# Spare matmuls on zeros between attention levels, and a reordered start, in a fused recurrence and two-layer expert kernel

## What is computed

```python
for t in range(S):
    kt, vt, rt, wt = (k[:, :, t], v[:, :, t], r[:, :, t], w[:, :, t])
    cur = np.einsum('bhd,bhe->bhde', u[None] * kt, vt)
    y[:, :, t] = np.einsum('bhd,bhde->bhe', rt, state + cur)
    state = wt[:, :, :, None] * state + np.einsum('bhd,bhe->bhde', kt, vt)
...
h = x @ w_in
g = np.where(pos, h, np.where(neg, 0.0, (h + beta) ** 2 / (4.0 * beta)))   # layer 1
g = np.where(h > 0.0, h, alpha * (np.exp(np.minimum(h, 0.0)) - 1.0))       # layer 2
return (g @ w_out)
```

## Time and profile before

| | |
|---|---|
| median of 3 runs | 1022.77 us (1022.32 to 1023.42) |
| profiled execution, own time | 1023.31 us |
| its span (first to last instruction) | 1021.5 us |
| PE busy | 989.6 us, 97% |
| DVE / ACT / POOL busy | 554.2 / 517.4 / 46.7 us |
| chain that ended last | PE 90%, DVE 4%, POOL 2% |

### The profile page before, as it was taken

One profiled execution on the slowest core, in us unless ns is written; L12 is line 12 of the kernel. 1 busy time (PEld: TensorE's weight loads), 2 busy tenths in 40 slices (PEclk: granted clock), 3 DMA queues, 4 the chain that ended last, 5 costly groups with the idle time before them and its releaser, 6 DMA issues.

```text
span 1021.5 us, 25102 instructions
## 1 busy us (share of the span) xinstructions
PE 989.6 (97%) x11080; PEld 812.3 (80%) x11080; DVE 554.2 (54%) x824; ACT 517.4 (51%) x926; POOL 46.7 (5%) x44
## 2 busy tenths in 40 slices
PE   4799899999999999999999999999999999999998
PEld 4788888777777777787778888888888888888886
DVE  5687877667666766776643454433433333333332
ACT  3465356454635354545456775554445444444543
POOL 5830000000000000000000000000000000000000
PEclk9899999999999999999999999999999999999999
DMA  9622032032002203020206000000000001000000
GB/s 327 200 79 96 24 121 110 3 141 78 33 28 115 80 33 115 28 80 33 95 1 216 1 31 31 32 21 11 32 31 1 31 32 31 31 1 1 31 1 31
DMA packets 24699, 61.71 MB, mean 60 GB/s; under 512 B 2448, under 2 KB 6928, under 8 KB 24592
## 3 DMA queue, kind: packets, MB, share of 16 engines
q1 hardware_dynamic: 24592, 60.12, 16.7%
HBM read 50.68 MB, written 9.44 MB: 59 GB/s over the span
## 4 chain that ended last, share of the span: by engine, by line
PE 90%; DVE 4%; POOL 2%; issue 1%; ACT 1%; DMA 1%; SPq 0%; ACTq 0%; DVEq 0%; POOLq 0%
PE down_banks L576 39%; PE up_bank L576 29%; PE g_banks L576 17%; PE y_bank L576 3%; DVE att L1025 1%; POOL win_lo L515 1%; PE y_bank L628 1%; DMA scratch<-w_in_dram 1%; PE y_bank L710 1%; POOL r_nat L525 0%; DVE r_nat L1054 0%; DVE att L1007 0%; DVE att L1037 0%; DVE ynat L1075 0%; DVE ynat L1078 0%
## 5 line engine op out<-in xcount | busy, mean ns | idle before, releaser
L576 PE MATMUL down_banks<-g_hi,wout_lo 128*128 128x512 f32 (+1 forms) x624 | 246.1, 394 | 0.0
L576 PE MATMUL down_banks<-g_hi,wout_hi 128*128 128x512 f32 (+1 forms) x624 | 235.9, 378 | 0.0
L576 PE MATMUL down_banks<-g_lo,wout_hi 128*128 128x512 f32 (+1 forms) x624 | 235.5, 377 | 0.0
L821 ACT CAST g_hi<-scratch 128x512 fp32r<-128x512 f32 (+1 forms) x192 | 116.0, 604 | 188.8 <-PE down_banks L576 118.9
L1096 DVE TENSOR_TENSOR g_lo<-scratch,g_hi 128x512 fp32r<-128x512 f32 (+1 forms) x192 | 128.4, 669 | 108.6 <-ACT g_hi L821 107.0
L576 PE MATMUL up_bank<-x_hi,win_lo 128*128 128x512 f32 (+1 forms) x480 | 182.6, 380 | 3.0 <-DVE g_lo L1096 1.8
L576 PE MATMUL up_bank<-x_lo,win_hi 128*128 128x512 f32 (+1 forms) x480 | 179.5, 374 | 0.0
L576 PE MATMUL up_bank<-x_hi,win_hi 128*128 128x512 f32 (+1 forms) x480 | 179.4, 374 | 0.0
L576 PEld LDWEIGHTS down_banks<-g_hi,wout_lo 128*128 128x128 f32 x624 | 117.8, 189 | 23.6
L576 PEld LDWEIGHTS down_banks<-g_hi,wout_hi 128*128 128x128 f32 x624 | 117.9, 189 | 23.3
L576 PEld LDWEIGHTS g_banks<-att 64*64 64x64 f32 (+1 forms) x5184 | 105.5, 136 | 36.2 <-issue 20.5
(11 more groups left out here) (98 smaller groups left out, 1075.6 us busy)
## 6 DMA issues: line engine op xcount, KB each, us to landing
att<-rT_dram SPq DMA_DIRECT2D x12, 512.0 KB, 4.0
att<-kT_dram SPq DMA_DIRECT2D x12, 512.0 KB, 5.6
att<-wT_dram SPq DMA_DIRECT2D x12, 512.0 KB, 6.5
r_nat<-rN_dram SPq DMA_DIRECT2D x12, 384.0 KB, 6.7
k_nat<-kN_dram SPq DMA_DIRECT2D x12, 384.0 KB, 7.7
att<-vN_dram SPq DMA_DIRECT2D x12, 384.0 KB, 6.9
x_dram<-r_nat SPq DMA_DIRECT2D x18, 256.0 KB, 2.3
ynat<-x_dram SPq DMA_DIRECT2D x6, 768.0 KB, 4.3
```

Source lines behind the costliest of these rows:

```text
L576: return nc.tensor.matmul(out, lhsT, rhs, start=start, stop=stop, **kw)
L821: return nc.scalar.copy(out, in_)
```

## The change

Five things, all in the first 60 us of the program:

- TensorE: 16 spare matmuls on a zeroed tile (128 rows, 256 columns, float32r) ahead of level 0 of group 0, then 11, 11, 9, 9, 9, 9 and 4 after its seven levels, and 3, 5 and 8 around the two `turn_x`. They write a PSUM place that nobody reads until slot 1 overwrites it. VectorE clears the tile first.
- VectorE: in group 0 of chunk 0 the mask of level l - 1 comes after the update of level l.
- GpSimd: `times_keys(0)` and `times_bonus(0)` after three weight pieces instead of six, `diagonal_output(0)` after six instead of nine and without its wait for them, `times_keys(1)` behind it.
- Pieces 6 to 8 get a buffer of their own (`extra`) in place of `ynat`, so that `diagonal_output` may write `ynat` sooner and pieces 19 and 20 no longer wait for piece 8.
- ScalarE: a one-column copy right at the start. A scratch area of the transfers is made smaller (memory for `extra`).

```diff
-STAGE = ["g0", "g1", "q", "scores0", "scores1", "scores2", "y0", "y1", "y2",
+STAGE = ["g0", "g1", "q", "scores0", "scores1", "scores2", "extra0", "extra1", "extra2",
...
-STAGED_BEHIND = {**{i: 5 for i in range(9, 14)}, 18: 2, 19: 8, 20: 8, 22: 16, 23: 17, 24: 18, 25: 22, 26: 23, 27: 21}
+STAGED_BEHIND = {**{i: 5 for i in range(9, 14)}, 18: 2, 22: 16, 23: 17, 24: 18, 25: 22, 26: 23, 27: 21}
+IDLE_AFTER_LEVEL = (11, 11, 9, 9, 9, 9, 4)
...
+        extra = sb("extra", [P, 3, TOK])
...
+        table_loaded = sb("table_loaded", [P, 1])
+        idle_work = x_lo[1][:, 0, 0:TH]
...
-                pool.wait_ge(w1_lo_ready, 9 if g == 0 else 21)
+                if g == 1:
+                    pool.wait_ge(w1_lo_ready, 21)
...
-            for i in range(6):
+            for i in range(3):
                 lo_of_weights(i)
             times_keys(0)
             times_bonus(0)
-            times_keys(1)
-            for i in range(6, 9):
+            for i in range(3, 6):
                 lo_of_weights(i)
             diagonal_output(0)
-            for i in range(9, 14):
+            times_keys(1)
+            for i in range(6, 14):
                 lo_of_weights(i)
...
+            def keep_busy(n):
+
+                for _ in range(n):
+                    mm(up_bank[1][:, 0:TH], idle_work[:, 0:P], idle_work)
+
+            pe.wait_ge(idle_work_ready, 1)
+            keep_busy(16)
             for l in range(NL):
                 pair_products(0, 0, l)
+                keep_busy(IDLE_AFTER_LEVEL[l])
             for b in range(2):
                 attend(0, b)
             turn_k(0, 0)
-            for b in range(2):
-                turn_x(0, b)
+            keep_busy(3)
+            turn_x(0, 0)
+            keep_busy(5)
+            turn_x(0, 1)
+            keep_busy(8)
...
             act.wait_ge(consts_ready, 1)
+            copy(table_loaded[:, :], consts[:, 0:1])
...
+            nc.vector.memset(idle_work.bitcast(F32), 0.0).then_inc(idle_work_ready, 1)
...
                 update(0, 0, l)
-                mask(0, 0, l)
+                if l:
+                    mask(0, 0, l - 1)
                 next_decays(0, 0, l)
```

More of the change, by code:

```diff
@@ L139, in build @@
                    **{f"scores_{i}": a_[1][:, i * DM:(i + 1) * DM] for i in range(5)},
-                   **{f"y{i}": ynat_flat[:, i * TOK:(i + 1) * TOK] for i in range(3)},
+                   **{f"extra{i}": extra[:, i, :] for i in range(3)},
                    **{f"y_{i}": ynat_flat[:, (2 + i) * DM:(3 + i) * DM] for i in range(2)},
@@ L193, in build @@
         consts_ready = sem("consts_ready")
+        idle_work_ready = sem("idle_work_ready")
         scores_zeroed = [sem(f"scores_zeroed{g}") for g in range(2)]
@@ L1244 @@
     arrays = {n: np.ascontiguousarray(a) for n, a in arrays.items()}
-    nc = bacc.Bacc("TRN2", target_bir_lowering=False, num_devices=1)
+    nc = bacc.Bacc("TRN2", target_bir_lowering=False, num_devices=1, dynamic_dma_scratch_size=8192)
     args = [nc.dram_tensor(n + "_dram", a.shape, mybir.dt.from_np(a.dtype), kind="ExternalInput").ap()
```

## The result

Over all its runs the changed kernel took 1027.45 us (median; 1023.22 to 1030.27), the kernel before, on the same chips, 1023.11 us (1021.36 to 1025.73): a ratio of 1.0044, 95% interval 1.0033 to 1.0056. It is slower by 4.3 us, by more than the 0.2% that can be told from no change, and lies above the range of the prediction. The profiled execution took 1029.1 us with a span of 1027.3 us.

The account below looks back on a forecast made before the run. The first 52 us decide, through group 1's first mask (the gate), held by GpSimd; -0.4 (mask) and -0.4 (clock) on profiled 1023.3 gave 1022.5, or 1022.0 against the median. Own range 1020.3 to 1024.0; with rivals 1018.8 to 1026.2.

Parts of the forecast that it names:

- update 5 starts at 23.2: VectorE, group 0's early levels: at 2.4 GHz with later masks, update 5 starts at 23.2 us instead of 23.9.
- the clock as a gain of 0.4: TensorE, low clock of 48.81 to 52.22 us: 0 to 1.5 us gained, 0.4 taken.
- the 0.4 at the gate: First mask of group 1 (the gate) on VectorE: starts at 39.1 us, 0.4 before 39.50.
- Part 1: TensorE, early levels: spare matmuls, if the clock rises, save 0.8 us per level of 64 products (1.93 to 1.14).
- Part 2: VectorE, group 0: later masks make TensorE wait for update and mask in series, eating nearly all the clock gives.
- Part 3: GpSimd queue: waits 3.5 us at diagonal_output until 26.1; score area clear at 39.0 us, not 36.87.
- Part 4: Slot 0 near 32.7 us, but group 1's first mask waits for the score area: 39.1; TensorE idles some 4 us.
- Part 5: From group 1's first mask to 52 us: neighbouring GpSimd operations 0, clock 0.4 us gained.
- B: TensorE's clock rises only at level 1 or 2: group 1's first mask at 41.7, total 1024.6 us; chance 0.23.
- C: TensorE's clock stays low through all seven levels: group 1's first mask at 44.5, +5.0, 1027.8 us; chance 0.12.
- D: GpSimd does not hold group 1's first mask: 3.6 to 4.2 us gained there, 1018.9 us; chance 0.18.
- E: The change does nothing (zeros don't count as work, masks hidden): 1022.8 us; chance 0.05.

Follow-up runs that it names:

- the third execution: The changed kernel, unedited, in the second of two further profilings: 1025.80 us.
- the first execution: The changed kernel's original profiled execution, unedited: 1029.1 us, span 1027.3 us.
- before's other execution: The kernel before, unedited, profiled once more for its clock record: 1021.75 us.
- the two edits aimed at it: Against the changed kernel: half as many spare matmuls, 512 columns wide (1026.68 us); loads of pieces 14 to 18 moved behind 9 to 13 (1027.96 us).
- masks back: Against the changed kernel: first group's masks put back behind their own level's update; 1025.10 us, ratio 1.0010.
- 512 wide: Against the changed kernel: half as many spare matmuls, each 512 columns wide; 1026.68 us, ratio 1.0031.
- loads later: Against the changed kernel: loads of weight pieces 14 to 18 moved behind those of 9 to 13 in SyncE's queue; 1027.96 us, ratio 1.0044.
- spare matmuls alone: Against the kernel before: only the spare matmuls and their cleared tile added; 1023.41 us, ratio 1.0000.
- GpSimd's order back: Against the changed kernel: GpSimd's queue returned to its order of before, the rest kept; 1024.27 us, ratio 1.0009.

## Why the prediction was wrong

Two steps failed: "update 5 starts at 23.2" in parts 2 and 3, and the clock as a gain of 0.4 in part 5. A third term, the 0.4 at the gate in part 4, was taken against an execution with a late gate of its own.

**Part 1 (spare matmuls)** was right in mechanism and size: 1.14 us per level from 5.82 on, 0.8 us each. What it took for granted, that a clock once up stays up through seven levels, held in one of three profiled executions. In the others it fell at 22.25 and at 14.25.

**Part 2 (masks)** was right: steps of 3.84, 3.84, 3.23 and 2.84 us in the third execution against the forecast 3.78, 3.78, 3.21 and 2.71.

**Part 3 (GpSimd)** had the mechanism and the lengths (12.87 us from sums to cleared area), and mis-sized one term: the wait of 3.5 us measured 7.17, 6.10 and 3.91. The failed step is "update 5 at 23.2", the best case of a number that the clock and TensorE's stop only make larger. Where that term came out nearly right (23.66), the execution still took 1025.80, so it isn't the only one. Everything late there arrives at the gate, one for one: from the third execution to the first the last update moves by 3.22 us and the gate by 3.21.

**Part 4** forecast the gate at 39.1 and measured 42.66, 40.90 and 39.45. The memset releases the mask, as forecast. TensorE idles 3.77 and 4.47 us in two of the executions, and 2.19 in the first. Slot 0 started at 39.35, 35.29 and 34.54 instead of 32.7; in the first execution TensorE's second stop and the low clock of 32.49 delayed the outputs (first one 34.44). The gain of 0.4 was taken against 39.50, a gate that the low clock had made late. Against the 37.71 of before's other execution even the forecast 39.1 is a loss of 1.4 us. The late slot cost nothing more, since the gate is GpSimd's. Nor did the later loads, which the prediction put at nothing: no engine waits for a transfer between 22 and 66 us in the three executions.

**Part 5** failed in sign. It bounded the clock's effect by 0 to 1.5 us of gain and took 0.4. It named the idle spell and the fall of the clock, and then took a gain of 0.4 all the same. It is a loss: 10.2 to 13.7 us at 1.2 GHz in all three executions instead of 3.4, and 22.3 to 22.8 us from gate to next chunk instead of 21.4 and 21.7, so 0.6 to 1.4 us. Filling the spell gave 21.1. The prediction has no term for a fall of 10 us; the two in the trace of before had lasted 6.83 and 3.41. The longer low stretches are not the profiled executions' alone: over the changed kernel's 20 executions the mean recorded clock has a median of 0.991, over the 95 of before beside the experiments 0.996.

**The rivals.** B (clock up only at level 1 or 2, mask at 41.7, 1024.6) is closest to what happens, with gates of 40.90 and 42.66, but its clock came up early and fell later. It also had part 5's gain of 0.4. C was measured by taking the spare matmuls out: gate 44.16 against 44.5, and +6.0 against +5.0. D was refuted: GpSimd holds the gate in every profiled execution of the changed kernel. A gate before 37 came only with GpSimd's order changed once more (36.32 and 36.13), and then the median was 1021 to 1022, not 1018.9. E was refuted by the products of 1.14 us.

**The sum.** Undoing one part at a time gives 2.3 us for the masks and 3.3 for GpSimd's order, and -1.7 for the spare matmuls, 3.9 together of the 4.3 measured. By the ratios the three are 3.5, 3.6 and -0.8, so each is known to 1 or 2 us, and since masks and order act through the same wait they needn't add up. The forecast had given the masks and the clock against each other (0), and GpSimd's order nothing beyond its 0.4 gain at the mask. Its own range doesn't come out of its terms either: with 1.4 and 1.0 us for the neighbours and 0 to 1.5 for the clock, 1022.0 becomes 1019.5 to 1023.4, not 1020.3 to 1024.0; the measured time lies above both.

**What stays open.** How much of part 5's loss is the idle spell's own (above). Whether the stop at level 4 costs anything in the median: the two edits aimed at it lie at +3.6 and +4.7 around +4.3, and two of the changed kernel's own three executions had none. Why the instruction packet of that block starts at 20.07 us in one execution and at 16.88 in another, with TensorE at the same place to 0.01 us from level 2 on. Whether the loads have a part in it isn't shown. The short fall near 108 to 121 us (1.5 us or so) came in the first and the third execution of the changed kernel, and in some others of the kernels tried, the two fastest among them, but in neither of before; whether the change makes it likelier wasn't settled.

## What to carry to other kernels

An operation that waits in a queue holds up all behind it, so put it where its input arrives in the usual execution, not in the best one, and ask who waits for the work behind it. Before buying speed for a stretch, check in the chain that the stretch is on it: here 1.5 us won in the levels were worth nothing, since the outputs waited for GpSimd anyway. Where a change opens an idle spell of TensorE just ahead of critical work, price the clock behind that spell as a possible loss, and try filling it. And before setting a forecast against one profile, see what its own clock did: a low stretch in it can pass for a gain of the change.

## What the hardware showed unexpectedly

- After TensorE had idled 3.77 to 4.73 us ahead of the products behind the gate, the clock was at 1.2 GHz for 10.2 to 13.7 us in four executions of three kernels (changed twice, masks back, 512 wide) and for 6.8 in one (loads later), though TensorE was busy again. The idle spell alone doesn't set the length: with spells of 2.2 to 2.4 us it was 3.41 (before), 6.83 (spare matmuls alone, GpSimd's order back) and 10.24 (changed, first execution).
- With spare matmuls of 256 or 512 columns the clock was up from somewhere between 4 and 20 us on; with twice as many of 128 columns and TensorE busy throughout, level products stayed at 1.93 us through levels 0 to 4, and 2.4 GHz came at 51.76.
- The changed kernel had the clock up from between 4.0 and 5.2 us on in three executions, but it fell again at 22.25, 14.25 and 42.73.
- TensorE stood up to 2.09 us with no engine or data to wait for, at every place a multiple of 256 instructions from the others, and went on 2.2 to 3.0 us after a 16 KB instruction packet had started; most often the same places were passed without a stop.
- An update that reads its decays from PSUM took 1.22 us in every profiled execution at levels 2 to 5 of the first group, while those of group 1 with both inputs in SBUF took 1.76 and 1.77 next to GpSimd's work (43.79 and 48.37). The Trainium skill (SBUF — State Buffer, "Who interferes with whom") has two SBUF inputs as the condition for being blocked; these rows agree with the condition and with a full block. Each of the two updates, and before's of 2.63 us at 44.65, ends 1.08 us behind the end of the GpSimd operation that ran when it started (44.46, 49.06 and 46.20), and the GpSimd operations that start during the two take 1.99 and 2.80 us instead of 1.0 and 1.81. What an update loses goes with how much is left of the other's operation: 0.5 us here, 1.4 for the one at 44.65.
